# One-tile expert loop with single buffers, row scaling moved to GpSimd, and gathers spaced by a wait

## What is computed

```python
def _moe2_ref(x, w_gate, w_noise, noise, w1, w2):
    N, D = x.shape                       # 1536, 512
    E = w_gate.shape[1]                  # 8
    noisy_logits = x @ w_gate + np.log1p(np.exp(x @ w_noise)) * noise
    top2 = np.argpartition(-noisy_logits, 2, axis=1)[:, :2]
    ...
    for e in range(E):
        for k in range(2):
            mask = top2[:, k] == e
            ...
            h = np.maximum(x[mask] @ w1[e], 0.0)
            out[mask] += top2_w[mask, k, None] * (h @ w2[e])
    return out.astype(np.float32)
```

## Time and profile before

| | us |
|---|---|
| median of 3 runs | 794.21 (793.56 to 794.41) |
| the profiled execution, its own time | 792.93 |
| its span, first to last instruction | 791.3 |
| granted TensorE clock, mean | 0.985 |

### The profile page before, as it was taken

One profiled execution on the slowest core, in us unless ns is written; L12 is line 12 of the kernel. 1 busy time (PEld: TensorE's weight loads), 2 busy tenths in 40 slices (PEclk: granted clock), 3 DMA queues, 4 the chain that ended last, 5 costly groups with the idle time before them and its releaser, 6 DMA issues.

```text
span 791.3 us, 12870 instructions
## 1 busy us (share of the span) xinstructions
PE 766.0 (97%) x4116; PEld 644.9 (82%) x4117; DVE 303.6 (38%) x827; ACT 233.6 (30%) x539; POOL 440.9 (56%) x252
## 2 busy tenths in 40 slices
PE   7999999999999999999799999999999999998994
PEld 6777899899889899898678888888888888886873
DVE  4777543235323522444763233222332222221224
ACT  5999522223223222322211121111211111211114
POOL 6888995001200200069598494798849898933031
PEclk8999999999999999999999999999999999999997
DMA  8642492000100200063631521616161616125037
GB/s 274 240 137 93 137 372 79 1 1 14 66 1 0 80 0 0 0 218 104 241 114 41 208 85 50 255 40 252 40 254 51 241 51 252 40 76 163 27 97 263
DMA packets 37279, 92.12 MB, mean 116 GB/s; under 512 B 5760, under 2 KB 5888, under 8 KB 37248
## 3 DMA queue, kind: packets, MB, share of 16 engines
q1 hardware_dynamic: 22416, 45.83, 17.0%
q0 software_dynamic: 10368, 37.75, 13.3%
q10 hardware_dynamic: 4464, 8.13, 2.8%
HBM read 67.06 MB, written 24.64 MB: 116 GB/s over the span
## 4 chain that ended last, share of the span: by engine, by line
PE 92%; DVE 2%; another core or an unknown queue 2%; issue 2%; ACT 1%; POOL 1%; DVEq 0%; POOLq 0%; ACTq 0%
PE bank L1502 21%; PE bank L1477 21%; PE bank L1336 17%; PE bank L1386 17%; PE bank L1289 4%; PE bank L1486 3%; PE bank L1280 3%; PE bank L1262 2%; PE bank L1463 2%; PE bank L1402 1%; PE bank L1396 1%; ACT arena L731 1%; DVE arena L992 1%; DVE gathered_a L1246 0%
## 5 line engine op out<-in xcount | busy, mean ns | idle before, releaser
L1502 PE MATMUL bank<-ring,hidT_hi 128*128 (+1 forms) x496 | 161.5, 407 | 4.7 <-issue 3.9
L619 POOL TENSOR_TENSOR ring<-ring_raw,ring 128x2048 fp32r<-128x2048 f32 x32 | 148.0, 4626 | 2.5
L665 POOL DMA_INDIRECT sorted_x<-y_rows,arena x24 | 24.0, 1001 | 206.8 <-DVEq L1043 200.7
L1477 PE MATMUL bank<-ring,xsT_hi 128*128 (+1 forms) x496 | 137.4, 399 | 1.1 <-DVE xsT_lo L1091 0.8
L617 POOL TENSOR_TENSOR ring<-ring_raw,ones 128x2048 fp32r<-128x2048 f32 x32 | 115.9, 3622 | 22.4 <-DMA ring_raw<-in_moe_w 22.4
L1386 PE MATMUL bank<-w_out_sb,gated_hi 128*128 128x512 f32 x384 | 120.8, 395 | 0.0
L1502 PEld LDWEIGHTS bank<-ring,hidT_hi 128*128 128x128 f32 x496 | 93.1, 193 | 25.6 <-issue 5.1
L1477 PEld LDWEIGHTS bank<-ring,xsT_hi 128*128 128x128 f32 x496 | 91.3, 189 | 19.3 <-issue 1.9
L1502 PE MATMUL bank<-ring,hidT_lo 128*128 (+1 forms) x248 | 99.4, 401 | 0.0
L1336 PE MATMUL bank<-xT_hi,w_in_hi 128*128 (+1 forms) x256 | 87.1, 340 | 0.0
L1336 PE MATMUL bank<-xT_lo,w_in_hi 128*128 (+1 forms) x256 | 86.2, 337 | 0.0
(11 more groups left out here) (186 smaller groups left out, 1096.4 us busy)
## 6 DMA issues: line engine op xcount, KB each, us to landing
ring_raw<-in_moe_w POOLq DMA_DIRECT2D x24, 1024.0 KB, 9.3
ring_raw<-in_moe_w SPq DMA_DIRECT2D x8, 1024.0 KB, 6.8
xs<-sorted_x SPq DMA_DIRECT2D x31, 256.0 KB, 2.7
sorted_y<-ys ACTq DMA_DIRECT2D x31, 256.0 KB, 2.0
sorted_y<-zeros SPq DMA_DIRECT2D x1, 4864.0 KB, 26.4
arena<-in_k SPq DMA_DIRECT2D x8, 520.0 KB, 4.0
w_in_raw<-in_moe_w_in SPq DMA_DIRECT2D x2, 2048.0 KB, 10.2
arena<-in_q SPq DMA_DIRECT2D x8, 384.0 KB, 3.2
```

The lines of the kernel that those rows point to most:

```text
L619: ins = pool.tensor_tensor(lo, raw, hi.bitcast(F32), ALU.subtract)
L665: pool.indirect_dma_start(out=sorted_x[:, :], out_offset=bass.IndirectOffsetOnAxis(ap=row_at[k][:, kk:kk + 1], axis=0), in_=y_rows_all[:, ...
L1477: last = pe.matmul(bank[1 + half][:, :], x[u][:, c * P:(c + 1) * P], ring[:, bass.ds(at * 2 * WE + (w + c * FE + half * BANK), BANK)], sta ...
L1502: last = pe.matmul(bank[5][:, :], x[:, c * P:(c + 1) * P], ring[:, bass.ds(at * 2 * WE + (w + CH * FE + c * DM), DM)], start=c == 0 and n ...
```

## The change

- **One tile, single buffers.** `xs`, `xsT_hi`, `xsT_lo`, `ys` have one buffer each, and the loops of PE, DVE, ACT and SP have a body of one tile. SP loads tile t + 1's rows when tile t's have been turned (before: when tile t - 1's had). DVE copies a result to `ys` when the store of the result before has landed (before: of the one two tiles back). At the loop's head `turn_rows(1)` stands behind `up(0)`, and its copies on ACT and DVE behind `relu_out(0)`.
- **Scaling.** POOL multiplies `gathered_a` by the gate values, between the two series; ACT's 12 multiplications are gone.
- **Spacing.** Each gather from the third of its series on waits until the gather two places ahead of it has landed.
- DVE's small table that splits the stores by parity is replaced by one instruction.

```diff
@@ sync (SP)
             sp.wait_ge(scattered, 16 * TOP * KB * (NBLK - 1))
-            for u in range(2):
-                load_rows(first * CAP + u * P, u)
+            load_rows(first * CAP)
 ...
             sp.wait_ge(y_ready, NBLK * KB)
+            sp.wait_ge(xs_turned, 1)
+            load_rows(first * CAP + P)
 ...
-            with sp.Fori(0, (TILES - 3) // 2) as it:
-                for u in range(2):
-                    t = 2 * it + 2 + u
-                    start = tile_start(t)
-
-                    sp.wait_ge(scattered, 16 * TOP * TT)
-
-                    sp.wait_ge(xs_turned, t - 1)
-                    load_rows(start, u)
 ...
+            with sp.Fori(2, TILES) as t:
+                start = tile_start(t)
+
+                sp.wait_ge(scattered, 16 * TOP * TT)
+
+                sp.wait_ge(xs_turned, t)
+                load_rows(start)
@@ gpsimd (POOL)
-                for u in range(2):
-                    pool.wait_ge(ys_stored[u], stores[u])
+                pool.wait_ge(ys_stored, stores)
                 for i in range(TT):
+                    if i >= 2:
+                        pool.wait_ge(gathered[kk][i - 2], 16)
                     pool.indirect_dma_start(
                         out=rows[:, i, :], out_offset=None, in_=sorted_y[:, :],
                         in_offset=bass.IndirectOffsetOnAxis(ap=ordered[kk][:, i:i + 1], axis=0),
                     ).then_inc(gathered[kk][i], 16)
+                if kk == 0:
+                    pool.wait_ge(gates_ready, 2)
+                    for i in range(TT):
+                        pool.wait_ge(gathered[0][i], 16)
+                        pool.tensor_tensor(gathered_a[:, i, :], gathered_a[:, i, :],
+                                           gate_at[0][:, i:i + 1].to_broadcast([P, DM]), ALU.mult).then_inc(scaled, 1)
@@ scalar (ACT)
-            rows_turned_out(1, 1)
             relu_out(0)
+            rows_turned_out(1)
             hid_turned_out(0)
 ...
-            act.wait_ge(gates_ready, 2)
-            for i in range(TT):
-                act.wait_ge(gathered[0][i], 16)
-                act.mul(gathered_a[:, i, :], gathered_a[:, i, :], gate_at[0][:, i:i + 1]).then_inc(scaled, 1)
@@ vector (DVE)
                 if not first:
 
-                    dve.wait_ge(ys_stored[u], 8 * (t - u))
-                dve.tensor_copy(ys[u], bank[5][:, :]).then_inc(ys_ready, 1)
+                    dve.wait_ge(ys_stored, 16 * t)
+                dve.tensor_copy(ys[:, :], bank[5][:, :]).then_inc(ys_ready, 1)
@@ tensor (PE)
-            turn_rows(1, 1, 16)
-            up(0, 0, known=True, ranks_of=NBLK - 1)
+            up(0, known=True, ranks_of=NBLK - 1)
+            turn_rows(1)
             turn_hidden(0)
 ...
-            with pe.Fori(2, (TILES - 3) // 2) as it:
-                for u in range(2):
-                    t = 2 * it + u
-                    up(t, u)
-                    turn_rows(t + 1, 1 - u, 16 * (it + 1 + u))
-                    down(t - 1)
-                    turn_hidden(t)
 ...
+            with pe.Fori(2, TILES - 1) as t:
+                up(t)
+                turn_rows(t + 1)
                 down(t - 1)
                 turn_hidden(t)
```

More of the change, by code:

```diff
@@ L310, in build @@
         hidT_lo = place_at("hidT_lo", hidT_at + FE, [FE], F32R)
-        ys_all = place_at("ys", X_LO, [2, DM])
-        ys = [ys_all[:, u, :] for u in range(2)]
+        ys = place_at("ys", X_LO, [DM])
         behind_rows = X_LO + KB * DM
[L315 to L321, removed]
+        xs = place_at("xs", behind_rows, [DM])
+        hid = place_at("hid", behind_rows + DM, [FE])
+        xsT_at = behind_rows + DM + FE
+        xsT_hi = place_at("xsT_hi", xsT_at, [DM], F32R)
+        xsT_lo = place_at("xsT_lo", xsT_at + DM, [DM], F32R)
+        assert xsT_at + 2 * DM <= X_LO + PAIRS * S
         sorted_x = nc.dram_tensor("sorted_x", (E * CAP, DM), F32, kind="Internal").ap()
@@ L381, in build @@
         down_split = sem("down_split")
-        xs_loaded = [sem(f"xs_loaded{u}") for u in range(2)]
+        xs_loaded = sem("xs_loaded")
         xs_turned = sem("xs_turned")
@@ L393, in build @@
         ys_ready = sem("ys_ready")
-        ys_stored = [sem(f"ys_stored{u}") for u in range(2)]
+        ys_stored = sem("ys_stored")
         gathered = [[sem(f"gathered{kk}_{i}") for i in range(TT)] for kk in range(TOP)]
@@ L863, in _, with tile @@
             act.activation(gate_e[:, :], gate_d[:, :], ACT.Exp).then_inc(route_act, 1)
[L865 removed]
+            def tile(t, more):
                 relu_out(t)
                 if more:
[L868 removed]
+                    rows_turned_out(t + 1)
                 hid_turned_out(t)
[L870 to L876, removed]
[L879 to L882 removed]
+                store_rows(t - 1)
+            with act.Fori(1, TILES - 1) as t:
+                tile(t, True)
+            tile(TILES - 1, False)
             act.wait_ge(expert_done, TILES + 1)
[L885 to L887 removed]
+            act.wait_ge(ys_stored, 16 * (TILES - 1))
+            act.copy(ys[:, :], bank[5][:, :]).then_inc(ys_ready, 1)
+            store_rows(TILES - 1)
         @block.vector
@@ L1225, in _, with tile @@
             dve.sem_inc(gates_ready, 1)
-            with dve.Fori(0, (TILES - 5) // 2) as it:
-                for u in (1, 0):
-                    t = 2 * it + 4 - u
-                    relu_out(t)
-                    rows_turned_out(t + 1, 1 - u)
-                    result_out(t - 1, 1 - u)
-                    hid_turned_out(t)
-            for t in range(TILES - 2, TILES):
+            def tile(t, more):
                 relu_out(t)
-                if t < TILES - 1:
-                    rows_turned_out(t + 1, 1 - t % 2)
-                result_out(t - 1, 1 - t % 2)
+                if more:
+                    rows_turned_out(t + 1)
+                result_out(t - 1)
                 hid_turned_out(t)
+            with dve.Fori(3, TILES - 1) as t:
+                tile(t, True)
+            tile(TILES - 1, False)
             for i in range(TT):
@@ L1476, in up @@
                         for half in range(2):
-                            last = pe.matmul(bank[1 + half][:, :], x[u][:, c * P:(c + 1) * P],
+                            last = pe.matmul(bank[1 + half][:, :], x[:, c * P:(c + 1) * P],
                                              ring[:, bass.ds(at * 2 * WE + (w + c * FE + half * BANK), BANK)],
```

80 lines of the change are left out of this document (30 added, 50 removed).

## The result

The changed kernel took 790.83 us (median of 7 runs, 789.21 to 791.61); the kernel before took 794.41 us beside it (7 runs, 791.32 to 796.94). The ratio is **0.9947**, 95% interval 0.993 to 0.9964. The profiled execution took 789.44 us with a span of 787.8, against 792.93 and 791.3 before. The forecast was 789.3, that is 4.9 us less than before; measured are 3.6 us less in the medians and 3.5 in the spans.

What follows compares the result with a forecast made beforehand. PE bounds the kernel (92% of the chain), with 5.3 us lost to late signals. Head +0.7, signals -5.3, second series from 757.1 for 25 us, end 786.4: -4.9 on the 794.21 median gives 789.3 us, range 784.6 to 797.

Steps and rivals of the forecast that it cites:

- The late signals go, -5.3 us: Expert loop under the first gather series: spacing stops PE's signals reaching ACT and DVE late, returning 5.3 us.
- Rival (1): PE's late signals stay as long as before; 794.6 us, no change; chance 0.18 together with waits that don't bind.
- Spacing, pair of gathers 3.95 us: POOL's gather series: two gathers take landing 3.1 plus restart 0.85 us, instead of 2.5; first series lands after 24.1.
- Series b in 25 us: Second gather series, sharing DMA engines with the stores: 25 us from start to last landing, 757.1 to 782.1.
- The bound of 4.2 us for a landing: Slow case for gathers: landings take 4.2 us, as stores to out did; a series then lasts 30.7 us.
- The end: forecast 786.4: Kernel's end: last sum 783.0, its store lands some 3 us later, 0.4 follow; 786.4 against 791.3, -4.9 us.
- The loop's head, +0.7: Start of the expert loop: up(1) waits for turn_rows(1) behind up(0), starting at 393.2 instead of 392.50.
- Single buffers, 0: Steady expert loop: row loads and result stores stay covered by a tile of 12.40 us; cost 0.
- Scaling on POOL, 0: Between the gather series: 12 multiplications of 1.34 us, 16 us in all, fit POOL's idle time; price 0.
- Rival (3): DVE's sums hold back second-series gathers, making it 3.4 us longer; 792.7 us; chance 0.13, shared with signals late by half.
- rival (2): Signals stay late until a series ends; PE loses another 6.9 us, +7, 801 us; chance 0.19.
- Rival (4): POOL finds each gather landed, series as before, late signals stay, no change; chance 0.18, shared with signals staying late.

Runs made afterwards that it cites:

- e9: The changed kernel without the spacing waits, run on a chip where the kernel before has late signals; 0.9993 of the kernel before, span 791.3 us.
- e10: The kernel before plus only the spacing waits in both gather series, on a chip where the kernel before has late signals; 0.9965 of it, span 787.8 us.
- e1: The kernel before plus only the spacing waits in both gather series, on a chip without late signals; 1.0052 of the kernel before, span 788.0 us.
- e11: The changed kernel, with SP issuing no store to out before the last gather of the second series has landed; span 791.8 us.
- e6: The changed kernel again, unedited, on a second chip; 0.9944 of the kernel before.
- e4: The changed kernel without the spacing waits, on a chip without late signals; 0.9989 of the kernel before, span 783.1 us.
- e5: The kernel before again, unedited, on a second chip, where late signals showed; 0.9981 of the kernel before.
- e2: The kernel before with only the scaling moved from ACT to POOL; 1.0012 of the kernel before, span 783.2 us.
- e3: The kernel before with spacing waits and POOL scaling, keeping its two-tile loops and double buffers; 1.0081 of the kernel before, span 788.1 us.
- e7: The changed kernel with spacing waits in the first gather series only, the second issued dense; 0.9914 of the kernel before.
- e12: The changed kernel with the second gather series waiting three places back instead of two, the first unchanged; 0.9914 of the kernel before, 787.36 us median.
- e8: The changed kernel with each gather waiting for the one three places ahead instead of two, in both series; 0.9911 of the kernel before.

## Why the prediction came out right, point by point

- **The late signals go, -5.3 us: right where they exist.** Tiles stay 12.4 us apart and series b starts at 756.55, forecast 757.1. e9 and e10 show that the waits do it. But I took the rows of one profile for a property of the kernel, and it is one of kernel and chip: on chip A the same step is worth nothing and the waits cost 0.5% (e1). That the number came out is in this part luck: on chip A it would have been a loss. A rival with that content was missing. Rival (1) had the late signals stay as a price; it had no place for a chip that has none to lose.
- **Spacing, pair of gathers 3.95 us: the sum was right, its terms were off against each other.** A landing took 3.4 us in the early pairs, not 3.1; POOL started 0.26 us after it, not 0.85. The first pairs of series b are 3.63 us; series a's five are 3.77 on average ((725.63 - 706.78) / 5), its last two gathers start 1.58 us apart, not 1.27, and it took 24.0 us, forecast 24.1. The 0.85 was from a wait for PE, and I had no row of a wait for a DMA's landing in POOL's list just ahead of a gather. The Trainium skill, "DMA: Bandwidth & Descriptors", section "Anatomy of one DMA — SWDGE (gpsimd) path", gives figures by which a landing would take an estimated 2.6 us; the fastest of the changed kernel's series b took 3.4, and the measurement decides.
- **Series b in 25 us: too short by 3, the term that was mis-sized most.** I gave 0.9 us more than series a for sharing the DMA engines with the stores. e11 measures that share at 2.9 us, and 25.1 us is what series b takes without them. The bound of 4.2 us for a landing was passed too: 5.4.
- **The end: forecast 786.4, measured 787.38 (the last landing) and the span 787.8.** The last landing of series b came 2.5 us later than forecast (784.6 for 782.1), and the last store landed 2.0 us after its sum instead of 3: the misses offset each other in part, and 1.4 of the 4.9 us forecast did not come.
- **The loop's head, +0.7: it depends on the clock.** Before, the granted clock was 1.00 in 379 to 384 us and 0.50 in 388 to 391; in the first profile of after it was the reverse (windows, before):

```profile
379.00:384.00 5.00, 4.58 (x22) 3.50 (x21) 4.31 (x3) 1.98 (x5) 4.60 (x1) 1.00 1.03 403
388.00:391.00 3.00, 2.96 (x8) 1.85 (x7) 2.31 (x14) 0.00 (x1) 0.00 (x0) 0.50 0.00 0
```

  and after:

```profile
379.00:384.00 5.00, 5.00 (x15) 4.13 (x16) 3.27 (x2) 1.82 (x4) 4.68 (x2) 0.50 1.03 410
388.00:391.00 3.00, 2.75 (x17) 2.07 (x16) 2.14 (x14) 1.07 (x2) 0.00 (x0) 1.00 0.00 0
```

  Where the 1.2 GHz stretch lies ahead of PE's wait for the routing (until 387.5), that wait swallows it; behind it, it lies on the path. This is no effect of the edit: e1 and e10 are one kernel, and one shows 0.50 and the other 1.00 in 388 to 391. With like clocks the edit's price can be read, counted from the end of that wait. At 0.50, `up(1)` starts 5.0 us after it before (387.49 to 392.50) and 6.1 in e6 (387.44 to 393.57): +1.1 us. At 1.00, it is 4.5 us both in e10 (387.83 to 392.36) and in the first profile of after (387.66 to 392.18): nothing. PE's timeline of e6:

```profile
393.57 1.27 PE L1456 MATMUL bank<-ring,xsT_hi 128*128 128x512 f32 x4
```

  ACT's, the copy that this `up(1)` waited for:

```profile
392.11 0.59 ACT L835 CAST xsT_hi<-bank 128x512 fp32r<-128x512 f32 x1 [0.26 <-PE bank L1442]
```

  and PE's of e10:

```profile
392.36 1.17 PE L1479 MATMUL bank<-ring,xsT_hi 128*128 128x512 f32 x4
```

  The forecast of +0.7 was made from a trace with the clock at 0.50 there, and was 0.4 short for that clock: it had the copy at 391.60, and it began at 392.11.
- **Single buffers, 0: right.** e4 and e9 (changed kernel, dense) are at 0.9989 and 0.9993 of before, and the trace of the changed kernel names no wait of PE for `xs`. In e9, though, series b starts at 765.6, 2.5 us later than in e5; its `turn_hidden` under series a comes round after 19.1 us, against 17.6. Whether the buffers or the place of PE's gaps do that isn't shown, and its total time is that of before all the same.
- **Scaling on POOL, 0: right.** Twelve took 12.02 us (1.0 each, forecast 1.34) and ended at 740.2; e2 measured no change.
- **Rival (3), sums hold gathers: true, and small.** Four of series b's gathers took 1.35 us instead of 0.96, at 770.23 to 778.07, each begun some 0.24 us behind the start of a sum. That is 4 x 0.39 = 1.6 us at most, half of what I gave the rival, and only the part on the chain counts. The Trainium skill, "SBUF — State Buffer", section "Who interferes with whom", calls the shared ports an exclusive lock; the gathers that begin beside a sum agree in kind. The gather at 767.70, which ran beside sums too, took 0.95 and does not.
- **Rival (1), the signals stay late,** and **rival (2), late until the series ends:** neither happened with two gathers in flight. **Rival (4), the waits don't bind:** ten of ten bound in series a.

**What stays open.** Why PE's signals reach ACT and DVE late under dense gathers; the runs show when, not by what way. Since PE itself falters in the same stretches, it is not only the way from PE to the other two. Transfers of instructions by DMA don't go with it: from 706 to 727 us the kernel before and e5 show none and have late copies, e4 shows one and has no late copy. Why one chip of three showed none: each chip was used in one sitting, so chip and time are not told apart. The changed kernel itself was not run on chip A; e1 and e3, its spacing in the other loop, let me estimate that it would lose 0.5 to 0.8% there. Whether e7 or e12 keep any gain on chip A wasn't tried.

## What to carry over

A stall that the chain of waits can't name and that stands in one profile may belong to the chip or the moment: before an edit is built on it, profile the unchanged kernel on a second one. Spacing these gathers by waits on their landings took such stalls away, but each pair of gathers then lasts as long as a landing and the next start; do it where the series has slack (series a landed 36 us before the first sum) and leave the series that ends the kernel dense. A transfer series that overlaps stores must be priced with the landings of that mix, not with those of the quiet stretch.

## What was unexpected of the hardware

- One kernel, with dense gathers, had PE's signals 8 us late on one chip and on time on another: a span of 791.3 against 783.1 us (e9, e4). On a third the kernel before has them late too (e5).
- In such a stretch PE itself starts one weight load or matmul every 0.7 us and waits for nothing that the trace names (e5, 722.89 to 725.71).
- The delay of ACT's first copy under series a grows with the gathers in flight: 0 with two, 4.0 us with three, 7.9 and 8.2 with no limit (e6, e8, e5, e9).
- POOL starts a gather 0.26 us after the landing that it waited for, where it took 0.85 us from PE's signal to the start of its DMA. The kind of signal isn't the reason: the first gather of series b starts 0.77 us after the landing of the store that it waits for (755.78 to 756.55 in the changed kernel).
- A stretch of some 3 us or more at a granted clock of 0.50 lies before or behind the same wait of PE in different executions of one kernel, and moves the head of the loop by 0.5 us in the old order (5.1 in e1, 4.5 in e10, from the end of that wait) and by 1.6 in the new one (6.1 in e6, 4.5 in the first profile of after).
